# Attention and two feed-forward layers on one core: the first loads on two queues, and one weight split moved ahead on GpSimd

## The reference

```python
# attention: q, k, v are (4, 8, 576, 64); each query sees itself and the 63 keys before it
scores = q @ k.T / sqrt(64); masked outside the window; attn = softmax(scores); out = attn @ v
x = out as (2304 tokens, 512)
# first layer, d_ff 1536
xn = x / sqrt(mean(x*x) + 1e-6) * rms_g
g = xn @ w_gate; x = (g * sigmoid(g) * (xn @ w_val)) @ w_out
# second layer, d_ff 2048
h = x @ w_in; r = maximum(h, 0); y = (r * r) @ w_out2
```

## Time and profile before

| | |
|---|---|
| median of three executions | 911.52 us (909.70 to 911.78) |
| the profiled execution | 909.82 us, of which the span is 907.9 |
| TensorE (PE) busy | 889.4 us, 98% |
| VectorE (DVE) busy | 609.4 us, 67% |
| GpSimd (POOL) busy | 583.8 us, 64% |
| ScalarE (ACT) busy | 483.5 us, 53% |
| granted TensorE clock | 1.00 |

### The profile page before, as it was taken

One profiled execution on the slowest core, in us unless ns is written; L12 is line 12 of the kernel. 1 busy time (PEld: TensorE's weight loads), 2 busy tenths in 40 slices (PEclk: granted clock), 3 DMA queues, 4 the chain that ended last, 5 costly groups with the idle time before them and its releaser, 6 DMA issues.

```text
span 907.9 us, 14817 instructions
## 1 busy us (share of the span) xinstructions
PE 889.4 (98%) x5356; PEld 879.4 (97%) x5356; DVE 609.4 (67%) x861; ACT 483.5 (53%) x872; POOL 583.8 (64%) x568
## 2 busy tenths in 40 slices
PE   6999899999999999999999999999999999999998
PEld 6998899999999999999999999999999999999998
DVE  7777777767867766867776767767377675577222
ACT  4887755654466463555554445544355453455332
POOL 7897749967368977347868448573368553485332
PEclk9999999999999999999999999999999999999999
DMA  9995122211222212222222122222422221420122
GB/s 236 249 230 150 45 64 70 70 53 59 82 65 71 70 53 60 69 80 72 70 70 58 58 88 71 65 58 70 138 72 71 62 67 59 157 70 18 59 70 93
DMA packets 105944, 76.99 MB, mean 85 GB/s; under 512 B 24464, under 2 KB 88976, under 8 KB 105872
## 3 DMA queue, kind: packets, MB, share of 16 engines
q1 hardware_dynamic: 105872, 76.05, 29.1%
HBM read 71.31 MB, written 4.72 MB: 84 GB/s over the span
## 4 chain that ended last, share of the span: by engine, by line
PE 82%; POOL 9%; issue 3%; ACT 3%; DVE 3%; DMA 0%; SPq 0%; POOLq 0%; ACTq 0%; DVEq 0%
PE bank L618 26%; PE bank L620 25%; PE bank L619 25%; PE bank L570 2%; PE bank L593 2%; POOL h L490 1%; POOL sq L529 1%; POOL h L501 1%; POOL w_raw L439 1%; POOL wide L460 1%; POOL w_raw L435 1%; POOL probs L466 1%; PE bank L579 1%; ACT w_hi L816 1%; ACT acts L816 0%
## 5 line engine op out<-in xcount | busy, mean ns | idle before, releaser
L618 PE MATMUL bank<-xc_hi,w_hi 128*128 128x384 f32 x844 | 283.8, 336 | 2.1 <-ACT acts L816 1.0
L620 PE MATMUL bank<-xc_hi,w_lo 128*128 128x384 f32 x844 | 282.1, 334 | 0.0
L619 PE MATMUL bank<-xc_lo,w_hi 128*128 128x384 f32 x844 | 282.1, 334 | 0.0
L618 PE MATMUL bank<-hs_hi,d_hi 128*128 128x384 f32 x672 | 225.3, 335 | 1.9 <-POOL d_lo L508 1.9
L619 PE MATMUL bank<-hs_lo,d_hi 128*128 128x384 f32 x672 | 224.6, 334 | 0.0
L620 PE MATMUL bank<-hs_hi,d_lo 128*128 128x384 f32 x672 | 224.6, 334 | 0.0
L508 POOL TENSOR_TENSOR d_lo<-d_raw,d_hi 128x512 fp32r<-128x512 f32 x84 | 127.1, 1513 | 146.0 <-ACT d_hi L816 146.0
L1219 DVE TENSOR_TENSOR hs_lo<-h,hs_hi 128x768 fp32r<-128x768 f32 x84 | 85.5, 1018 | 126.4 <-ACT hs_hi L816 126.2
L618 PEld LDWEIGHTS bank<-xc_hi,w_hi 128*128 128x128 f32 x844 | 158.4, 188 | 5.8 <-issue 1.8
L619 PEld LDWEIGHTS bank<-xc_lo,w_hi 128*128 128x128 f32 x844 | 158.5, 188 | 0.0
L620 PEld LDWEIGHTS bank<-xc_hi,w_lo 128*128 128x128 f32 x844 | 158.4, 188 | 0.0
(11 more groups left out here) (92 smaller groups left out, 1257.4 us busy)
## 6 DMA issues: line engine op xcount, KB each, us to landing
d_raw<-in_w_down SPq DMA_DIRECT2D x48, 256.0 KB, 2.6
w_raw<-in_w_gate SPq DMA_DIRECT2D x36, 256.0 KB, 2.9
w_raw<-in_w_val SPq DMA_DIRECT2D x72, 128.0 KB, 2.8
d_raw<-in_w_out SPq DMA_DIRECT2D x36, 256.0 KB, 2.6
w_raw<-in_w_in SPq DMA_DIRECT2D x24, 256.0 KB, 2.7
w_raw<-in_w_in SPq DMA_DIRECT2D x48, 128.0 KB, 2.6
k_sb<-in_kT SPq DMA_DIRECT2D x16, 288.0 KB, 4.3
q_diag<-in_qT SPq DMA_DIRECT2D x32, 144.0 KB, 4.9
```

The source lines that it names most:

```text
L618: pe.matmul(ps, w_h, v_h, start=first, stop=False, skip_group_check=joined)
L619: pe.matmul(ps, w_h, v_l, start=False, stop=False, skip_group_check=joined)
L620: return pe.matmul(ps, w_l, v_h, start=False, stop=last, skip_group_check=joined)
```

## The change

Two separate edits. The loads of sequence 0 are issued by two engines instead of one, and the q loads are cut behind the first group's three blocks. SP issues the upper q, ACT the k and the lower q. k and the two first q pieces count on a new semaphore, `first_in` (48), for group 0; the two other pieces count on `qk_in[0]`, for which group 1 waits. In `slot`, the later waits on `qk_in[0]` are 16 lower, since its first round now brings 32. The second edit moves POOL's `down_low(M0[r])` in the last up step of each run from the end of the step to a place ahead of `h_b(u - 1)`.

```diff
+        first_in = sem("first_in")
+        def first_rows(row, blocks):
+            return qT[bass.ds(row, HD), :].rearrange("d (b c) -> d b c", c=WIN)[:, blocks, :]
 # SyncE
-            load_qk(0)
+            sp.dma_start(q_diag[0][0:WIN, 0:GU, 0:WIN], first_rows(0, slice(0, GU))).then_inc(first_in, 16)
+            sp.dma_start(q_diag[0][0:WIN, GU:NBLK, 0:WIN], first_rows(0, slice(GU, NBLK))).then_inc(qk_in[0], 16)
             load_qk(1)
 # GpSimd
                     if u + 2 < U0[q]:
                         weight_sum(u + 2, 0)
+                    if u == U0[q] - 1:
+                        down_low(M0[r])
                     if u > S0[r]:
                         h_b(u - 1, r)
...
                     if q < PAIRS and s == 9:
                         diagonals(q)
-                    if u == U0[q] - 1:
-                        down_low(M0[r])
 # TensorE, slot(g)
+                    if g == 0:
+                        pe.wait_ge(first_in, 48)
+                    elif g == 1 or g % GPS == 0:
+                        pe.wait_ge(qk_in[par], 48 * (seq // QR + 1) - (16 if par == 0 else 0))
                     if g % GPS == 0:
-                        pe.wait_ge(qk_in[par], 48 * (seq // QR + 1))
 # ScalarE, ahead of everything else
+            act.dma_start(k_sb[0][:], kT[0:P, :]).then_inc(first_in, 16)
+            act.dma_start(q_diag[0][WIN:P, 0:GU, WIN:P], first_rows(HD, slice(0, GU))).then_inc(first_in, 16)
+            act.dma_start(q_diag[0][WIN:P, GU:NBLK, WIN:P], first_rows(HD, slice(GU, NBLK))).then_inc(qk_in[0], 16)
```

## The result

The changed kernel is 0.18% faster: ratio 0.9982 (95% interval 0.9975 to 0.9989) against the kernel before. The medians are 909.04 us and 910.3 us, over 20 executions each; one execution of 3276.22 us is no part of the ratio. Forecast were 1.6 us less; the ratio says 1.6, the medians 1.3. The profiled execution took 909.08 us with a span of 907.1, 0.8 less than before's span of 907.9.

A forecast was written before the change was run, and what follows sets the result against it. TensorE, busy 98% of the span, was taken to bound the kernel, so only its waits could be won. Terms 0.63 and 0.96 summed to 1.6 us, taking the median from 911.52 to 909.9, range 907.9 to 911.8.

The forecast's parts named there:

- 0.63: First edit, at group 6: 0.28 us of slack plus 0.35 of filled transfer time won, bounds 0.28 and 0.99.
- 0.96: Second edit, last up steps: 0.80 us won where no rb copies stand, 0.08 in each of two with them.
- The pair of rows from the second chunk: Profile rows: hs_lo started together with d_lo takes 2.08 us and ends 0.81 after it, against 0.96 alone.
- the order of ScalarE's stream: Last up step: rb copies stand behind the gate waiting for ga, so they end at 197.07 instead of 196.61.
- ACT was forecast: Sign at the first down matmul where rb is copied: a 0.5 to 0.6 us wait put down to ACT.
- Runs 3 to 5: Second edit there: TensorE doesn't wait for d_lo, later needs are over 2 us away, cost put at nothing.
- The start: First matmul of group 0: near 4.7 instead of 5.86, 1.15 us earlier; 5.8 would refute it.
- the landing of the lower rest: ACT's third load, for group 1: today's third lands at 5.81, perhaps some tenths later, well ahead of 7.28.
- the central claim of the first edit: Group 6 is held by its own q load, so TensorE stands idle some tenths there near 14.3.
- The rival on the slower side: ACT's slow issues delay the lower rest, group 1 is 4.0 us late: 3.0 us slower, 914.6; chance 0.04.
- The fill of the transfer engines' idle share: Loads from 1.6 to 4.4 us: DMA share 0.80 rises towards 1.07, bounds 0 and 0.71 us, taken as 0.35.
- that rival: ACT loads its table ahead of the DMA issues, the first edit wins nothing: 0.96 us won, 910.6; chance 0.12.

The follow-up runs named there:

- dlow_only: Only the second edit (d_lo of the first chunk ahead of h_b), against the kernel before: ratio 0.9990.
- loads_sp_held: First edit alone, with SyncE also waiting for first_in before issuing sequence 1's loads, against the kernel before: one execution, 912.37 us at clock 0.998.
- loads_only: Only the first edit (loads of sequence 0 on two queues), against the kernel before: ratio 1.0000.
- both_best: Second edit, lower rest on SyncE, sequence 2's k and q before sequence 1's v, rb copies before the gate, against the kernel before: ratio 0.9967.
- loads_qk2_first: First edit with the lower rest on SyncE and sequence 2's k and q ahead of sequence 1's v, against the kernel before: ratio 0.9996.

## Why the prediction was right, and where it was wrong

The total of 1.6 us came out, but not as it was added up, and partly by luck. Of the two terms, 0.63 and 0.96, the first was nothing and the second carried all; and at equal clock the change won about 0.9 us. That the ratio says 1.6 all the same comes, as far as the times tell, from the nine of before's 20 executions that took 910.90 us and more.

The second edit, step by step as predicted, from the trace of dlow_only, whose last up product stands within 0.03 us of before's (196.41 and 196.44): end of `hs_lo` 194.81 predicted, 194.78 measured; `ga` 195.20 and 195.17; end of the `rb` copies 197.07 and 197.02; first down matmul 197.33 and 197.24. The pair of rows from the second chunk gave the size of the standstill, and the order of ScalarE's stream gave who is late next. Won were 0.14, 0.15 and 0.79 us instead of 0.08, 0.08 and 0.80. Both links are tested: with `hs_lo` free of `d_lo` the gap shrinks, with the copies moved it is gone. The profile itself names neither: it puts the gap down to "issue", where ACT was forecast. Runs 3 to 5 cost nothing, as forecast.

The first edit was put at 0.63 us, and brought nothing. The start was right (4.7 predicted, 4.77, 4.64 and 4.55 measured). The step that failed is the landing of the lower rest: "it may be some tenths later, still well ahead of 7.28". I took the landing of the old third load, 5.81, and named the neighbour, sequence 1's k, but gave it tenths. It landed at 6.9 and 7.6, with that k and more beside it on SyncE's queue; loads_sp_held shows the neighbours' price, 1.6 to 2.3 us. With that the head start was spent at group 1, which began 2.9 us behind the first matmul and not within 1.4, and the idle time at group 6 that was to bear out the central claim of the first edit stayed out: by its own sign the claim is refuted for the kernel as changed. The rival on the slower side had the place (the lower rest, group 1) but the wrong cause: ScalarE's issues are as short as SyncE's (0.63 us for the third), it is the sharing. The fill of the transfer engines' idle share, counted at 0.35 us, isn't seen either: from 1.6 to 4.4 us the changed kernel's DMA share is 0.75, against 0.80, and group 6's last load landed at 15.0 in it and at 13.9 in loads_only, against 14.66 before. The Trainium skill ("DMA: Bandwidth & Descriptors", section "Issuing engines are not separate DMA queues") says that issuing DMAs on several engines at once only saves the time of issuing. The trace agrees: the share didn't rise, and sequence 1's k was issued at 2.25 instead of 2.60, 0.35 us earlier (the prediction had 0.65). The table load stood behind the DMA issues, at 2.61, so that rival is out.

## What to carry to other kernels

Ahead of splitting a load over two queues, count what the freed queue will issue next to it: here a small transfer with a waiting consumer landed at 6.4 us ahead of the large ones on their own queue, and at 6.9 and 7.6 on a second queue beside them. A moved instruction is worth the distance to the next wait of the same consumer; list the consumer's waits in order, and follow each back through any engine that the moved instruction holds up. Here the moved `d_lo` alone won 1.3 us, and with a copy put into an idle hole ahead of a gate, 3.0 (both at clock 1.00). And before a difference of a microsecond is put down to an edit, see whether both kernels' executions were of the same kind.

## What else the runs showed of the hardware

Executions of one kernel came in two kinds, over a microsecond apart: before at mean clock 1.00 had 909.8 (27 of 33 executions in one session), at 0.998 it had 911.2 (4 of 33). Two more, at 0.999, took 909.81 and 910.32. The trace of both_best is of the second kind. TensorE first, in stretches of 2 us; the columns are as in the earlier trace rows:

```profile
108.00:110.00 2.00, 1.31 (x12) 1.15 (x11) 1.80 (x2) 1.88 (x7) 1.66 (x2) 1.00 0.00 0
110.00:112.00 2.00, 1.03 (x6) 0.87 (x5) 1.68 (x4) 1.95 (x5) 0.00 (x0) 0.88 0.00 0
112.00:114.00 2.00, 2.00 (x8) 2.00 (x7) 2.00 (x3) 1.05 (x2) 0.00 (x0) 0.50 0.03 8
114.00:116.00 2.00, 2.00 (x10) 2.00 (x10) 1.74 (x2) 0.62 (x1) 0.00 (x0) 0.77 0.01 3
```

The granted clock falls to 0.50, the 1.2 GHz level, for about 3 us at the seam, and matmuls of 384 columns stand 0.32 us apart instead of 0.17. Ahead of it TensorE had been idle twice, for 0.69 us until 109.39 and for 0.97 us until 111.26. The kernel before has nearly the same idle time there, and in its trace the clock stayed at 1.00:

```profile
108.00:110.00 2.00, 1.39 (x12) 1.16 (x10) 1.34 (x3) 1.91 (x5) 1.84 (x3) 1.00 0.00 0
110.00:112.00 2.00, 0.95 (x7) 0.81 (x7) 1.97 (x3) 1.90 (x6) 0.44 (x1) 1.00 0.00 0
```

How often it falls differed (0 of 11 executions of loads_only, 7 of 11 of loads_qk2_first); why was not tried. At 1.4 us from one kind to the other it is as large as the change studied here, and splitting the executions by their clock shows more than the medians do.
